# The dispatch of a long block in two halves, with a chunk of the next block between them

## The reference, cut to what matters

```
x = attention(q, k, v, mem_k, mem_v)          # 3072 tokens x 512
h = x @ w_in                                  # 512 -> 2048
g = h * sigmoid(h)
x = g @ w_out                                 # 2048 -> 512
logits = x @ phi                              # 32 slots
d = exp(logits - logits.max(0)); d /= d.sum(0)
slot_input = d.T @ x                          # 32 x 512, sum over all tokens
for e in range(8):                            # 4 slots an expert
    slot_out[e] = relu(slot_input[e] @ w1[e]) @ w2[e]
c = softmax(logits, axis=1)
out = c @ slot_out
```

## Time and profile before

| what | us |
|---|---|
| three executions: median (lowest to highest) | 461.74 (460.4 to 462.73) |
| the profiled execution, whole | 461.4 |
| its span, from the first to the last instruction | 459.4 |
| TensorE busy in the span | 442.7 |
| DVE busy | 272.7 |
| ACT busy | 138.7 |

### The profile page before, as it was taken

The page is one execution under the profiler, slowest core; times in us unless marked ns, Lnnn a source line. Parts: engine busy times, 40 slices in busy tenths (PEclk is TensorE's granted clock), DMA queues, the critical chain, the costliest instruction groups (busy, mean ns, idle before and its releaser), DMA issues.

```text
span 459.4 us, 12251 instructions
## 1 busy us (share of the span) xinstructions
PE 442.7 (96%) x5438; PEld 330.8 (72%) x5438; DVE 272.7 (59%) x528; ACT 138.7 (30%) x257; POOL 47.4 (10%) x44
## 2 busy tenths in 40 slices
PE   6899999999999999999999999999999999999982
PEld 5798877778876778768787777887678779543551
DVE  5677746948477656487584785655664548541133
ACT  2666343232431423223234314233122222210022
POOL 2775100101001001010010010010000000010000
PEclk9999999999999999999999999999999999999997
DMA  8998244023050050230321402226200589999988
GB/s 303 412 414 337 99 156 173 1 93 116 2 201 9 17 191 1 93 118 0 111 97 60 150 1 86 100 93 277 92 0 0 208 358 419 340 418 424 420 357 356
DMA packets 14819, 81.57 MB, mean 178 GB/s; under 512 B 1584, under 2 KB 1712, under 8 KB 8880
## 3 DMA queue, kind: packets, MB, share of 16 engines
q1 hardware_dynamic: 14768, 80.81, 45.5%
HBM read 74.51 MB, written 6.29 MB: 176 GB/s over the span
## 4 chain that ended last, share of the span: by engine, by line
PE 89%; DMA 8%; DVE 1%; issue 0%; ACT 0%; DVEq 0%
PE h_ps L327 59%; DMA unit<-w 5%; PE lpu_ps L344 4%; PE sx_ps L284 4%; PE lpu_ps L375 4%; PE o_ps L311 3%; DMA qk_sb<-qk 3%; PE pt_ps L297 2%; PE sx_ps L375 2%; PE pt_ps L311 2%; PE h_ps L1081 2%; PE o_ps L1061 1%; PE lpu_ps L385 1%; PE sx_ps L1018 1%; PE h_ps L1018 1%; PE o_ps L344 1%
## 5 line engine op out<-in xcount | busy, mean ns | idle before, releaser
L327 PE MATMUL h_ps<-x_odd,w_pair 128*128 128x512 f32 x576 | 137.6, 395 | 0.0
L601 DVE SCALAR_TENSOR_TENSOR gT<-gT,h_ps 128x512 f32<-128x512 f32 (+1 forms) x112 | 67.8, 605 | 108.4 <-ACT gT L462 108.0
L327 PEld LDWEIGHTS h_ps<-x_odd,w_pair 128*128 128x128 f32 x576 | 106.4, 188 | 29.4 <-issue 5.9
L462 ACT ACTIVATE gT<-h_ps 128x512 f32<-128x512 f32 (+1 forms) x112 | 60.1, 536 | 214.2 <-PE h_ps L327 211.8
L327 PE MATMUL h_ps<-x_even,w_pair 128*128 128x512 f32 x384 | 92.4, 395 | 0.0
L327 PEld LDWEIGHTS h_ps<-x_even,w_pair 128*128 128x128 f32 x384 | 70.7, 188 | 19.6 <-issue 5.0
L609 DVE STREAM_TRANSPOSE gB<-gT 128x512 f32<-128x512 f32 x80 | 54.1, 696 | 0.8
L327 PE MATMUL h_ps<-x_short,w_pair 128*128 128x256 f32 x384 | 50.8, 287 | 0.4 <-DVE x_short L591 0.3
L585 POOL TENSOR_TENSOR sc<-sc,row_stats 128x512 f32<-128x512 f32 (+1 forms) x24 | 24.9, 1036 | 254.0 <-DVE row_stats L579 254.0
L327 PEld LDWEIGHTS h_ps<-x_short,w_pair 128*128 128x128 f32 x384 | 47.3, 191 | 4.6 <-issue 2.3
L472 ACT COPY pt<-pt_ps 64x512 f32<-64x512 f32 x46 | 26.5, 577 | 0.8
(11 more groups left out here) (183 smaller groups left out, 401.4 us busy)
## 6 DMA issues: line engine op xcount, KB each, us to landing
unit<-w SPq DMA_DIRECT2D x29, 1024.0 KB, 9.1
qk_sb<-qk SPq DMA_DIRECT2D x24, 640.0 KB, 5.9
v_sb<-v SPq DMA_DIRECT2D x24, 512.0 KB, 4.8
out<-unit SPq DMA_DIRECT2D x6, 1024.0 KB, 5.7
w_stage<-w_in SPq DMA_DIRECT2D x4, 1024.0 KB, 10.7
unit<-w_outT SPq DMA_DIRECT2D x4, 1024.0 KB, 13.5
unit<-w_out SPq DMA_DIRECT2D x4, 1024.0 KB, 6.0
unit_gT<-w SPq DMA_DIRECT2D x2, 1024.0 KB, 13.7
```

The source lines that it names most:

```text
L327: last = nc.tensor.matmul(h_ps[k % 2][:, 0:TOKS[b]], w_pair[:, k // 2, w, kc, k % 2 * 128:k % 2 * 128 + 128], x[:, lo, kc, 0:TOKS[b]], sta ...
L462: nc.scalar.activation(gt_of(b, k), h_ps[k % 2][:, 0:TOKS[b]], ACT.Tanh, scale=0.5).then_inc(tanh_done, 1)
L601: nc.vector.scalar_tensor_tensor(out=gt_of(b, k), in0=gt_of(b, k), scalar=1.0, in1=h_ps[k % 2][:, 0:TOKS[b]], op0=ALU.add, op1=ALU.mult).t ...
```

## The change

The dispatch of block 5, which stands in block 6, is cut in two by the chunks of g. Half 1 (chunks 8 to 15, places 10 and 11) comes where the whole dispatch was, after h chunk 4. Half 0 (chunks 0 to 7, places 8 and 9) comes after h chunk 5. Each half has the same 64 matmuls with 256 columns in place of 512. Half 1 raises a semaphore of its own, `u_half`, half 0 raises `u_mm`. The loads into the places 10 and 11 wait for `u_half`. DVE's accumulations in the last block come one step later, in the steps 5 to 8, and chunks of block 6 are turned from step 5 on, two in each step until step 9. The other blocks are as before.

```
+TURNED_LAST = {0: (), 1: (), 2: (), 3: (), 4: (), 5: (0, 1), 6: (2, 3), 7: (4, 5), 8: (6, 7), 9: (8, 9)}
...
+        u_half = sem("u_half")
...
             pe.wait_ge(gb_done, NCH * (b + 1))
             pe.wait_ge(sc_done, units_scored)
             rounds = TOKS[b] // 128
+            if b == LAST - 1:
+                pe_dispatch_half(pe, b, 1, u_half)
+                return
...
+        def pe_dispatch_half(pe, b, half, done):
+
+            for r in range(TOKS[b] // 128):
+                for c in range(4):
+                    for i in range(4):
+                        j = 4 * r + c
+                        last = nc.tensor.matmul(u_ps[i][32 * c:32 * c + 32, 256 * half:256 * half + 256],
+                                                eB[32 * i:32 * i + 32, 32 * j:32 * j + 32],
+                                                gb_groups(b, i, j)[:, 8 * half:8 * half + 8, :],
+                                                start=(r == 0), stop=(r == TOKS[b] // 128 - 1))
+            last.then_inc(done, 1)
...
+                if b == LAST and k == DISPATCH_STEP + 1:
+                    pe_dispatch_half(pe, b - 1, 0, u_mm)
                 if k == DISPATCH_STEP:
                     pe_dispatch(pe, b - 1, FIRST[b + 1] + 4 if b < LAST - 1 else NUN)
...
-                if b == LAST and 0 <= k - DISPATCH_STEP < 4:
-                    dve_acc(dve, b - 1, k - DISPATCH_STEP)
-                for turned in TURNED.get(k, (k,)):
+                if b == LAST and 0 < k - DISPATCH_STEP <= 4:
+                    dve_acc(dve, b - 1, k - DISPATCH_STEP - 1)
+                for turned in (TURNED if b < LAST else TURNED_LAST).get(k, (k,)):
                     dve_gb(dve, b, turned)
...
-        places += [(14, h_mm, NCH * LAST + 4)] + [(i, u_mm, NB - 1) for i in (10, 11)]
+        places += [(14, h_mm, NCH * LAST + 4)] + [(i, u_half, 1) for i in (10, 11)]
```

## The result

The changed kernel took 463.76 us as the median of six executions (463.31 to 464.65), the kernel before 460.88 beside it. The ratio is 1.0054, with a 95% interval of 1.0032 to 1.0076: 2.5 us slower, between 1.5 and 3.5. That lies just over the bound of 0.5% that the prediction set for "no change", and inside its range. The profiled execution has a span of 461.5 us.

A forecast was written before the change was run, and what follows sets the result against it. TensorE's chain before 399 us was taken to set the end through the saturated load queue. Records 1.06 + tile shape 0.14 = 1.2 us, stream gain 0: 461.4 + 1.2 = 462.6, plus 0.3 for the median, 462.9; range 460.8 to 465.0 us.

The forecast's parts named there:

- no change: Whole kernel: a time within about 0.5%, 2.3 us (459.4 to 464.1 us), counts as the same; chance 0.83.
- The bound: Block 6: TensorE's work before 399 us sets the end one for one, through the load queue saturated from near 400.
- the landing of the last load: End of the load queue: landing before 444.3 us despite a later last dispatch would show the forecast's last step wrong.
- The gain: Loads into places 10 and 11: issued about 1.7 us earlier, winning 1.5 to 1.7 us of stream, worth 0 at the end.
- Rival 1: Load queue: the stream's gain is kept to the end; -1.7 us, 460.0 us; chance 0.08.
- The first way: Dispatch of block 5: factor 1.24 for 256-column records, from the nearest rows, adds 4.40 x 0.24 = 1.06 us.
- The second way: Dispatch rounds: 0.24 us beyond the columns' time, paid eight times in place of four, adds 0.96 us.
- rival 2: Both halves: weights wait for their tile's matmul and 256 columns don't cover issue; up to +4.4 us, 466.3; chance 0.06.
- rival 3: Both halves: a least spacing between records, 27 ns, makes each piece 3.5 us; +2.6 us, 464.5; chance 0.05.
- wrong in the first step: Either half of the dispatch: a piece taking over 3.3 us, where 2.6 to 2.9 us was forecast.
- The change of tile shape: TensorE between dispatch and h chunk: one additional shape change costs 0.14 us, with bounds 0 and 0.3.
- rival 4: h chunks 10 to 12: DVE becomes late and TensorE waits for g; at most +0.8 us, 463.7; chance 0.07.

The follow-up runs named there:

- the idle matmuls: Kernel before plus eight idle 128x128 matmuls after h chunk 5 of block 6, 1.79 us on the chain; ratio 1.0053 (1.0032 to 1.0073).
- the hole closed for nothing: Kernel before, block 5's dispatch reading only chunks 0 to 7 with unchanged matmuls, so places 10 and 11 are free earlier; ratio 0.9993 (0.9973 to 1.0014).
- the hole left open in the halved kernel: Changed kernel, but the loads into places 10 and 11 wait for the second half again; ratio 1.0057 (1.0036 to 1.0078).
- the kernel with two chunks: Changed kernel with two h chunks between the halves (half 0 after h chunk 6), DVE's part one more step later; ratio 1.0084 (1.0058 to 1.0109).

## Why the prediction came out as it did

**The bound: right in direction, not shown to be one for one.** What TensorE loses ahead of its last dispatch reaches the end: the idle matmuls passed their time on within the interval, and the loads behind the last dispatch went out 2.5 us later in the changed kernel, beside a time that is 2.5 us longer. But the prediction had the queue of loads alone carry it there. In the kernel before TensorE's own work behind the dispatch is only 1.2 us shorter than the queue, and in the changed kernel, as in the one with idle matmuls, the chain has no load at its end. The prediction had named the landing of the last load as its test, before or after 444.3: it landed 0.6 us after, where 1.2 us of delay were forecast and 2.5 us arose. In the profiles 1.4 of these 2.5 us are taken up before the last copy, and 1.05 us come back in the last stores. What part of that is scatter stays open.

**The gain: right.** The release came at 372.44 (predicted near 372.7), and no gain from the stream is seen. This was tried twice, with the hole closed for nothing (0.9993) and with the hole left open in the halved kernel (1.0057 beside 1.0054). Rival 1 falls at its price of 1.7 us; up to 1.2 us the first interval doesn't exclude. The holes' sum was predicted at some 5 us and was 5.3 before 401.5. The first hole closed by half only, not nearly whole: 0.8 us of it remain. That changed nothing.

**The bare price of the halves: right, by one of its two ways.** Predicted 1.06 us for the doubled records, measured 2 x 2.68 - 4.40 = 0.96, seen in the first half and again in the undisturbed second half of the kernel with two chunks (2.73). The first way, a factor of 1.24 from the nearest rows, came close by luck, since those rows don't hold the price of a record. The 1.07 us for 16 records of 256 columns were the first behind TensorE's wait for the last load; running on, 16 such records take 0.86 us, just as 8 of 512 do (this line is of the changed kernel):

```profile
427.06 0.86 PE lpu_ps L780 x16
```

In the logits each group pays one entry of 0.14 us, and 2 x 0.57 pays it twice: without it 16 records of 512 columns take 1.71 us and 16 of 256 take 0.86, the same per column. The second way holds: a round of the dispatch takes 0.24 us beyond its columns, paid eight times in place of four, and a round of a half takes 2.68/4 = 0.67 = 0.43 + 0.24. (Its words "at 2.4 GHz" don't give its 0.43 us: 512 columns at 2.4 GHz are 0.21 us. What gives 0.43 is rows 6, eight records in 0.86 us, four side by side.)

The mechanisms of the rivals 2 and 3 are out: a piece of 128 records ran in 2.68 us, so it has no floor near 25 ns a record, which would be 3.2 us. But by its own signs the prediction would have been sent to them. It called a piece of over 3.3 us "wrong in the first step", and the second took 4.28; rival 2 was to decide over 6.6 us for both, and they took 2.68 + 4.28 = 6.96; and rival 3 forecast 7.0 us for both and 464.5. Only the kernels that move or remove the stop tell the two causes apart. The change of tile shape, for which I took 0.14, can't be seen: the chunk between takes the same 1.63 us as before.

**The step that failed** is the sentence that TensorE's part of the sum was 1.06 + 0.14 = 1.2 us. It lacked a term. I counted the 256 additional instructions as work for the array and not as something that has to be brought in. The measured sum up to the last dispatch is 0.96 for the records, 1.60 for one stop while the next block of instructions comes, 0.16 for DVE's order, together 2.7 us, for a forecast of 1.2. The mechanism was missing, and that the range held the time is luck: its upper part was there for rival 3's dear records. The level helped too. The forecast of 462.9 was counted from a median of 461.74, while the kernel before took 460.88 beside the changed one, so that the time was missed by 0.9 us and the difference by 1.3. The sign was forecast rightly within the measurement's reach, but the larger chance was on "no change", and the time fell 0.04% over that bound.

What the runs show of that term: stops at the same instruction numbers (9,610 to 9,628 and 9,866 to 9,878 as counted, behind 4,648 and 4,776 matmul records in the profile) in six kernels, with five different pieces of work at these numbers; one stop put there on purpose in a kernel with the whole dispatch; a packet of the instruction queue 2.3 to 2.6 us ahead of the end of each; the same stop whether the queue of loads was full or nearly empty. What stays open is when a block is asked for. I held that a request waits for the end of a burst of short instructions. It goes out late in bursts (the packet comes at the start of the second half, not in the first), but in the kernel with 104 more instructions it came in the middle of a half, and the stock that I computed from the rule was wrong there. The rule is argued, the boundary is shown. That the stop is the wait for the packet's instructions is inferred too, from the packet ahead of each stop and the 16 KB; no run changes the fetch itself.

The Trainium skill has the block: the page Advanced Engine Details and Errata, section "ISA Cache", gives a line of 16 KB, or 256 instructions, and says that there are only two lines. The runs agree with the 256 (the packet of 16 KB, the distance of the stops). The same section names a larger cache for TensorE, which isn't seen: TensorE ran dry at a boundary less than 512 instructions after the packet before last. Had I looked for it, two bursts of 256 instructions 1.6 us apart would have been a rival.

**DVE (rival 4): a small part.** It isn't TensorE's lateness but the order, 0.16 us. With the halves two chunks apart it grows into the chain.

## What to carry to other kernels

Splitting a burst of small matmuls cost more here than its columns: count the instructions as well, and see whether the engine can be fed. A stop whose releaser is "issue" on an engine that waits for nothing is a hint to look at the instruction queue, and moving the same code by some dozen instructions tells whether the place in the stream or the work is to blame. And before a hole in a queue is closed, look at the next hole: what ends that one says whether the gain arrives. Look as well how long the engine waits for the last load in the end: more than that wait (1.2 us here) can't be won.

## What the runs showed of the hardware that I had not expected

TensorE takes its instructions in blocks of 256 (packets of 16 KB, stops 128 matmul records apart), and in nine stops of seven kernels it starts again 2.3 to 2.6 us after the block's packet shows up in the trace. A half of the dispatch uses up a block in 2.68 us, the whole dispatch in 4.40 us, so the one has next to no cover and the other has some.

A stop of 3 us was followed by a lower clock, and so cost more than itself. In the kernel with 104 more instructions these stages come after the stop of 3.02 us:

```profile
386.00:388.00 2.00, 0.00 (x0) 0.00 (x0) 0.00 (x0) 0.00 (x0) 0.00 (x0) 1.00 0.96 389
388.00:390.00 2.00, 1.96 (x24) 1.14 (x25) 1.22 (x3) 0.00 (x0) 0.00 (x0) 0.85 0.78 324
390.00:392.00 2.00, 2.00 (x12) 2.00 (x11) 0.21 (x1) 0.00 (x0) 0.00 (x0) 0.50 0.14 57
392.00:394.00 2.00, 2.00 (x15) 2.00 (x15) 1.57 (x4) 0.52 (x2) 0.00 (x0) 0.80 0.02 8
```

The granted clock is 0.50, which is 1.2 GHz, from about 389.4 to 392.8 us (worked out from the 0.85 and 0.80 on either side), and four chunks of h take 7.43 us in place of 5.95. With 64 instructions more it is 0.63 and 0.52 from 388 to 392 us, after the stop of 3.05 us. After the stops of 0.99 and 1.41 us it stayed at 1.00.
